# Another order of the four-pair start in an attention and two-layer feed-forward kernel

## The reference, cut to what matters

```
q_d, k_d, v_d = means over runs of 4 tokens            # 144 tokens a head
out_d     = softmax(q_d k_d^T / 8) v_d                  # then each row repeated 4 times
out_local = softmax(q k^T / 8 where |i - j| < 4) v      # a band of 7 keys for each query
x = (out_up + out_local) as 2304 tokens x 512
h = x @ w_in1;  x = max(0.01 h, h) @ w_out1
h = x @ w_in2;  return (h - tanh(h)) @ w_out2
```

## Time and profile before

| | us |
|---|---|
| median of three runs | 953.63 |
| lowest and highest | 953.53, 953.75 |
| the profiled execution, its own time | 953.53 |
| its span in the trace | 951.8 |
| PE busy | 939.1 (99%) |
| DVE, ACT, POOL busy | 541.2, 557.2, 403.1 |

### The profile page before, as it was taken

The page is one execution under the profiler, slowest core; times in us unless marked ns, Lnnn a source line. Parts: engine busy times, 40 slices in busy tenths (PEclk is TensorE's granted clock), DMA queues, the critical chain, the costliest instruction groups (busy, mean ns, idle before and its releaser), DMA issues.

```text
span 951.8 us, 19930 instructions
## 1 busy us (share of the span) xinstructions
PE 939.1 (99%) x7026; PEld 882.9 (93%) x7026; DVE 541.2 (57%) x1078; ACT 557.2 (59%) x1351; POOL 403.1 (42%) x343
## 2 busy tenths in 40 slices
PE   8999999999999999999999999999999999999998
PEld 7799999999999999999999989899899898898997
DVE  6755445534544554453236576776666766766764
ACT  4665546445446455463446687666666756756754
POOL 3685417327246155171533667332233233233232
PEclk9999999999999999999999999999999999999999
DMA  7875111210121121102004022000000000000000
GB/s 159 192 197 141 46 33 27 51 36 26 39 51 26 25 51 40 38 2 67 1 2 134 12 58 86 30 5 1 34 0 0 33 0 0 33 0 0 34 1 33
DMA packets 87797, 41.48 MB, mean 44 GB/s; under 512 B 60352, under 2 KB 81344, under 8 KB 87744
## 3 DMA queue, kind: packets, MB, share of 16 engines
q1 hardware_dynamic: 87744, 40.78, 16.3%
HBM read 36.04 MB, written 4.72 MB: 43 GB/s over the span
## 4 chain that ended last, share of the span: by engine, by line
PE 88%; ACT 3%; POOL 3%; DVE 2%; DMA 2%; issue 1%; SPq 0%; ACTq 0%; DVEq 0%; POOLq 0%
PE ph L538 13%; PE ph L539 13%; PE ph L540 13%; PE acc L567 7%; PE acc L568 7%; PE acc L569 7%; PE acc L614 6%; PE acc L615 6%; PE acc L616 6%; PE banks L427 2%; PE banks L464 2%; PE banks L451 1%; POOL g_lo L1149 1%; PE banks L420 1%; POOL w_lo_b L1156 1%
## 5 line engine op out<-in xcount | busy, mean ns | idle before, releaser
L1149 POOL TENSOR_TENSOR g_lo<-scratch,g_hi 128x384 fp32r<-128x384 f32 x96 | 125.6, 1309 | 257.8 <-ACT g_hi L741 257.8
L996 DVE TENSOR_TENSOR ph<-g,ph 128x288 f32<-128x288 f32 x128 | 59.0, 461 | 165.4 <-ACT g L755 164.7
L538 PE MATMUL ph<-x_hi,w_hi_a 128*128 128x288 f32 (+1 forms) x448 | 143.6, 321 | 0.4 <-DVE x_lo L978 0.2
L540 PE MATMUL ph<-x_hi,w_lo_a 128*128 128x288 f32 (+1 forms) x448 | 139.9, 312 | 0.0
L539 PE MATMUL ph<-x_lo,w_hi_a 128*128 128x288 f32 (+1 forms) x448 | 139.9, 312 | 0.0
L1128 POOL TENSOR_TENSOR in_lo<-w_whole,in_hi 128x512 fp32r<-128x512 f32 x64 | 82.4, 1287 | 134.7 <-ACT in_hi L721 133.9
L755 ACT ACTIVATE g<-ph 128x288 f32<-128x288 f32 x128 | 52.5, 410 | 136.3 <-PE ph L540 136.3
L1133 POOL TENSOR_TENSOR out_lo<-w_whole,out_hi 128x512 fp32r<-128x512 f32 x64 | 86.0, 1343 | 71.8 <-ACT out_hi L725 71.6
L1030 DVE SCALAR_TENSOR_TENSOR scratch<-scratch,ph 128x384 f32<-128x384 f32 x96 | 53.2, 554 | 108.6 <-ACT scratch L804 104.0
L803 ACT ACTIVATE scratch<-ph 128x384 f32<-128x384 f32 x96 | 46.8, 487 | 108.4 <-PE ph L540 106.9
L983 DVE TENSOR_TENSOR g_lo<-ph,g_hi 128x288 fp32r<-128x288 f32 x128 | 58.6, 458 | 59.2 <-ACT g_hi L741 59.2
(11 more groups left out here) (273 smaller groups left out, 2660.4 us busy)
## 6 DMA issues: line engine op xcount, KB each, us to landing
out_dram<-o_stage SPq DMA_DIRECT2D x18, 256.0 KB, 2.1
w_whole<-in_moe_w_in_dram SPq DMA_DIRECT2D x16, 256.0 KB, 4.2
w_whole<-in_moe_w_out_dram SPq DMA_DIRECT2D x16, 256.0 KB, 4.9
qn<-in_q_dram SPq DMA_DIRECT2D x26, 144.0 KB
kn<-in_k_dram SPq DMA_DIRECT2D x26, 144.0 KB
v4n<-in_v_dram SPq DMA_DIRECT2D x26, 144.0 KB
vw<-in_v_dram SPq DMA_DIRECT2D x26, 122.5 KB
scratch<-in_moe_w_in_dram SPq DMA_DIRECT2D x8, 256.0 KB, 2.8
```

The source lines that it names most:

```text
L538: pe.matmul(bank, whi, x_hi[:, c, 0:width], start=(c == 0), stop=False)
L540: last = pe.matmul(bank, wlo, x_hi[:, c, 0:width], start=False, stop=(c == CD - 1))
L996: dve.tensor_tensor(ph1[:, 1 - f % 2, 0:T1], g1[:, f % 2, :], ph1[:, 1 - f % 2, 0:T1], ALU.max)\
L1149: pool.tensor_tensor(g2_lo[:, f % 3, :], g2[:, f % 2, :], g2_hi[:, f % 3, :].bitcast(F32), ALU.subtract).then_inc(g_lo_done, 1)
```

## The change

The tables of exceptions of all four engines are changed, and the items between the steps are put at the beginning of a slot rather than behind a step. The order of the queues, from slot 4 on, comes out as follows (only what differs):

| engine | before | after |
|---|---|---|
| PE | B2 B3 A6; C2 C3 B6; D2 A14 D3 C6 D4 A15 B11 | B2 A6 B3; C2 B6 C3; D2 A14 C6 D3 A15 D4 B11 |
| ACT | C0 C1 A8; C3 B7 A11 D0 B8 A12; D3 C7 B11 C8 A15 B12; B14 D7 B15 | C0 A8 C1; C3 A11 B7 D0 A12 B8; D3 A15 B11 C7 B12 C8; B14 B15 D7 |
| ACT, items | D8 w0 C13 w1 D11 x0 C15 D13 x1 D15 x2 | D8 C13 w0 D11 C15 D13 w1 x0 x1 D15 x2 |
| DVE | B4 B5 A8 A9; C4 C5 B8 B9; D8 C12 D9 | B4 A8 B5 A9; C4 B8 C5 B9; D8 D9 C12 |
| DVE, items | D14 C16 D15 x0 x1 D16 x2 | D14 C16 x0 x1 D15 x2 D16 |
| POOL | A6 B6 A9 A10 B9; C6 C9 D6 C10 D9 D10 w0 w1 | A6 A9 A10 B6 B9; C6 C9 C10 D9 D10 D6 w0 w1 |

Here w0 and w1 are `split_kept(0)` and `split_kept(1)`, x0 to x2 the quarters of x. The dummy products stay with the same steps in the same number. No instruction is added or taken away.

```diff
-EARLY = 2
+KEPT_HI_SLOTS = (22, 26)
+KEPT_LO_SLOTS = (24, 27)
+FILL = {("a", 1): 2, ("a", 3): 2, ("b", 1): 1, ("b", 3): 2, ("c", 3): 2}
+X_HI_SLOTS = {27: (0, 1), 28: (2,)}
+X_LO_SLOTS = {27: (0, 1), 28: (2,)}
...
# PE
-            for step, s in batch0({(A, 6): (B, 3), (B, 6): (C, 3), (C, 6): (D4, 3), (A, 11): (C, 4), (A, 15): (D4, 4),
-                                   (B, 11): (D4, 4), (C, 15): (D4, 12), (C, 16): (D4, 14)}):
+            for _, step, s, i in batch0({(A, 11): (C, 4), (B, 11): (D4, 4), (C, 15): (D4, 12), (C, 16): (D4, 14)}):
...
# ACT
-            for step, s in batch0({(A, 8): (C, 1), (A, 11): (B, 7), (A, 12): (B, 8), (A, 15): (C, 8), (B, 11): (C, 7), (B, 12): (C, 8),
-                                   (D4, 7): (B, 14), (C, 15): (D4, 11)}):
-                attention(step, s, 0)
-                if (s, step) == (D4, 8):
-                    split_kept(0)
-                elif (s, step) == (C, 13):
-                    split_kept(1)
-                elif (s, step) == (D4, 11):
-                    split_first_x(0)
-                elif (s, step) == (D4, 13):
-                    split_first_x(1)
-                elif (s, step) == (D4, 15):
-                    split_first_x(2)
+            done = -1
+            for slot, step, s, i in batch0({(D4, 7): (B, 15), (C, 15): (D4, 11)}):
+                if slot != done:
+                    for c in X_HI_SLOTS.get(slot, ()):
+                        split_first_x(c)
+                if slot != done and kept_at(KEPT_HI_SLOTS, slot) is not None:
+                    split_kept(kept_at(KEPT_HI_SLOTS, slot))
+                done = slot
+                attention(step, s, i)
...
# DVE
-            for step, s in batch0({(A, 8): (B, 5), (B, 8): (C, 5), (C, 12): (D4, 8), (D4, 9): (C, 12),
-                                   (A, 15): (C, 14), (A, 16): (A, 15), (B, 15): (D4, 12), (B, 16): (B, 15),
-                                   (C, 15): (B, 16), (C, 16): (D4, 14)}):
-                attention(step, s, 0, 0, FIRST.index(s))
-                if (s, step) == (D4, 15):
-                    lo_of_first_x(0)
-                    lo_of_first_x(1)
-            lo_of_first_x(2)
+            done = -1
+            for slot, step, s, i in batch0({(C, 12): (D4, 9), (A, 15): (C, 14), (A, 16): (A, 15),
+                                            (B, 15): (D4, 12), (B, 16): (B, 15), (C, 15): (B, 16),
+                                            (C, 16): (D4, 14)}):
+                if slot != done:
+                    for c in X_LO_SLOTS.get(slot, ()):
+                        lo_of_first_x(c)
+                done = slot
+                attention(step, s, i, i, FIRST.index(s))
...
# POOL
-            for step, s in batch0({(B, 6): (A, 6), (D4, 6): (C, 9)}):
-                attention(step, s, 0)
-            for f in range(EARLY + 1):
-                split_kept(f)
+            done = -1
+            for slot, step, s, i in batch0({(D4, 6): (D4, 10)}):
+                if slot != done and kept_at(KEPT_LO_SLOTS, slot) is not None:
+                    split_kept(kept_at(KEPT_LO_SLOTS, slot))
+                done = slot
+                attention(step, s, i)
+            split_kept(EARLY)
```

More of the change, by code:

```diff
@@ L85, in two_scale_attention_and_feed_forward @@
     WHOLE = CF - KEPT
+    EARLY = len(KEPT_HI_SLOTS)
     assert D == QB and DM == CD * P and LP * RUN == S and NB * QB == S and PAIRS == 4 + 2 * MIXED
@@ L260, in batch0, with placed @@
         def batch0(behind):
-            def placed(at, s):
-                yield at, s
+            def placed(slot, at, s):
+                yield slot, at, s, 0
                 for (moved, step), place in behind.items():
                     if place == (s, at):
-                        yield from placed(step, moved)
+                        yield from placed(slot, step, moved)
             for slot in range(STEPS + 3 * BEHIND):
@@ L272, in batch0, with kept_at @@
                     if (s, at) not in behind:
-                        yield from placed(at, s)
+                        yield from placed(slot, at, s)
+        def kept_at(slots, slot):
+            return slots.index(slot) if slot in slots else None
         def later(f, tile, last):
@@ L636, in _ @@
             fill(8, ph1[:, 1, :])
-            fills = {(A, 1): 2, (A, 3): 2, (B, 1): 1, (B, 3): 2, (C, 3): 2}
-            for step, s in batch0({(A, 6): (B, 3), (B, 6): (C, 3), (C, 6): (D4, 3), (A, 11): (C, 4), (A, 15): (D4, 4),
-                                   (B, 11): (D4, 4), (C, 15): (D4, 12), (C, 16): (D4, 14)}):
-                attention(step, s, 0)
-                fill(fills.get((s, step), 0), ph1[:, 1, :])
+            for _, step, s, i in batch0({(A, 11): (C, 4), (B, 11): (D4, 4), (C, 15): (D4, 12), (C, 16): (D4, 14)}):
+                attention(step, s, i)
+                fill(FILL.get(("abcd"[FIRST.index(s)], step), 0), ph1[:, 1, :])
             for step in range(HEAD):
```

## The result

The changed kernel takes 959.66 us (median of four runs, 958.63 to 960.5) against 953.69: the ratio is 1.0062, 95% interval 1.0045 to 1.0080. It is slower, by 6.0 us; 957.4 was forecast, with 954.4 to 960.2 as the range. The four runs of before agreed within 0.3 us, those of after lie 1.9 us apart. The narrow spread of before did not last: in the 65 executions of it measured later, beside the experiments, it took 951.6 to 957.3 us and twice 964 us. The profiled execution of the changed kernel took 958.32 us, span 956.5: 4.8 us over that of before, one of the quicker ones.

What follows compares the result with a forecast made beforehand. PE bounds the kernel after 46.5 us, untouched; waits set the earlier part. 953.53 + 2.36 (-0.43 + 2.29 + 0.13 + 0.37) + 1.5 for one clock fall = 957.4 us, range 954.4 to 960.2.

Steps and rivals of the forecast that it cites:

- two falls or more: Rival: PE's clock falls at least twice, once right after the pause before `hidden1(0, 0)`; 958.9 to 960.5 us, chance 0.16.
- Step 1: PE, A6 before B3: A6 waits for DVE's L929, B's scores end later, DVE's B4 starts 0.54 us late.
- Step 2: DVE A8 before B5, POOL A9 before B6: POOL no longer delays L946 and L952; C3 leads by 1.6 us.
- Step 3: PE, B6 before C3: PE stands from 16.1 to 18.0 us; the lead at DVE's C4 is 1.4 us.
- Step 4: ACT, B7 behind A11: B's exponential waits for A11's eviction, DVE's B8 starts at 23.16; lead 0.7 us.
- Step 5: Around D4 on PE and ACT: C7 runs behind A15 and B11, DVE's C8 starts at 30.86, 0.4 us late.
- Step 6: DVE's D9, now ahead of C12, stands until POOL's product of D ends; POOL's D10 starts 0.43 us early.
- Step 7: POOL's D6 behind D10: weight blocks end later and delay DVE's low quarters; 2.29 us, plus 0.13 (D15) and 0.37 (x2).
- The clock: PE's clock falls to half around its pauses: one fall on C4's or D4's masks and scores, 1.5 us (0 to 4.5).
- no hold: Rival: POOL's weight blocks don't delay DVE's low quarters at the end of the start; 953.6 us, chance 0.13.
- faster: Rival: the 1.6 us lead at DVE's C3 survives, shown by C8 before 28.5 us; 951.3 us, chance 0.07.
- no fall: Rival: PE's clock does not drop to half on the critical path; 955.9 us, chance 0.24.

Runs made afterwards that it cites:

- after, again: The changed kernel, unaltered, measured and profiled a second time: 959.23 us against 953.75 for the kernel before, ratio 1.0066.
- B6 late alone: The kernel before with only POOL's three v sums of pair B moved from behind A6 to behind A10: 953.30 us against 953.81, ratio 0.9984.
- those with the dummies: The changed kernel plus dummy products on PE, seven behind C2 and eight ahead of `hidden1(0, 0)`: median 962.44 us, ratio 1.0072 to the kernel before.

## Why the prediction was right, and where it was off

The direction and the range held, and the profile shows the mechanism of the forecast: pauses of PE, exponentials queued behind evictions, the hold under the weight blocks. But the median is 2.3 us above the forecast and lies where the rival "two falls or more" had it (958.9 to 960.5, chance 0.16). The profile has two falls, the second in that rival's place. So the middle of the forecast was low, by two things: 0.7 us of waits ahead of D10, and too little time at half the clock.

- **Step 1** (A6 before B3): 0.54 us forecast, 0.93 measured (B4 at 15.47 for 14.54; A6 began at 11.93, not 11.78, and from there to the end of B's scores it took 3.51 us, not 3.27). Right in kind.
- **Step 2** (the hold of A goes): right. L948 0.17 and L954 0.20 us, C3 at 19.43 for 20.65, a lead of 1.2 where 1.6 was forecast.
- **Step 3** (PE waits for B5 before B6): the pause came, 1.62 us for 1.9. But C4 on DVE started at 23.40, 0.7 us late, where a lead of 1.4 was forecast. Of these 2.1 us the fall of the clock makes 1.37.
- **Step 4** (B7 behind A11): right. DVE waits 0.49 us before B8, and the single undoing of ACT's table gives 1.7 us of stretch back.
- **Step 5** (C7 behind A15 and B11): right. C8 waits 0.50 us for it. It starts at 32.84; 30.86 and one fall of 1.5 would be 32.36.
- **Step 6** (D9 under POOL's product of D): right in place (L954 1.05 us long, C14's pause 1.88 us), but D10 started at 40.34 where -0.43 + 1.5 on 38.57 gave 39.64. 0.7 us of this sum were missed: 0.4 of them in step 1; the rest is in steps 3 to 6 and isn't told apart. D8, which waits 1.22 us for ACT's D7, started at 37.45 where 35.3 and one fall gave 36.8.
- **Steps 1 to 6 together**: without a fall (after, again) it is 28.9 us from A's maxima to D10, 0.3 more than before, where the forecast had 0.4 less. B6 late alone in the kernel before makes it 25.4. So the gain from the hold of A is real, 3.2 us up to D10, and by difference the rest of the new order takes 3.5 us: more than all of it.
- **Step 7** (D6, the hold, x0 to x2): the term is 2.79 in the forecast (2.29 + 0.50) and 2.77 in the profile (10.63 - 7.86). The edit alone in the kernel before gives 2.74 and shows the cause. An agreement to 0.02 is luck, though: in the second profile, with its late fall, the piece is 4.4 us longer than before and the hold doesn't set it.
- **The clock**: one fall of 1.5 us on the path was taken. The one over C's scores costs 1.37 us (7.93 - 6.56), in the executions that have it. The second one of the first profile cost little: the last quarter waited for DVE and not for PE, and the part behind it is longer by 0.2 us, where the rival had 1.5. The low estimate is in the number and the length of falls: each of the nine profiles with the changed order on at least one of PE, DVE and ACT has one, five have two or three, and where it falls between 39 and 46 us it stays at half for 10 us and more, through the short products up to `hidden1`. Such long falls were not in the forecast. The granted clock of the timed executions fits: the changed kernel is at 0.996 in its quick ones (958.3, 958.6), at 0.993 or 0.994 in most and at 0.989 in its slowest (962.9).
- **A sign that failed**: "if the half clock lies on no scores, the time is 955.9". In the second profile it lies on none, and the time is 958.82: the late fall stretched step 7, and the waits ahead of D10 were 0.7 us more than forecast.
- **The rule of the Trainium skill weighed in the forecast** (TensorE: Matmul & The Clock Gate, Part 1) was right to be set aside: the clock did fall behind or in pauses of 1.3 to 3.0 us, though not in each execution, and once with no pause over 0.56 us in the 10 us before. **The rival "no hold"** is dead (0.41 us a quarter with POOL idle). **The rival "faster"** had its mark at C8 before 28.5 us; it came at 32.84. **The rival "no fall"** is 955.9; the two executions with a clock of 1.000 are those with the dummies, at 957.7 and 958.6.
- What I had wrong and the total didn't show: w1 "costs nothing". It makes POOL stand for 1.58 us right behind D6 once D6 is gone. So the terms don't add when taken away: D6 costs 2.3 us put into the kernel before, and taken out of the changed one it gives 0.6 us of stretch and nothing that the times show.

## What to carry to other kernels

When a start-up is bound by waits, carry each queue forward with the traced lengths and look at what stands ahead of each late item on every engine, the lightly busy ones too; that gave the place and the size of the largest term. Before an edit is undone to save its price, ask what is next in line: here it was w1 on ACT for POOL, and the slow clock for PE. And a pause of PE in a stretch of short products should be priced twice, once as the pause and once as the half clock that may follow it.

## What the runs showed of the hardware

- A DVE instruction with both inputs in SBUF, or a small scalar operation in SBUF, stood until a running POOL instruction was nearly over (2.98 us for 0.45; L954 1.05 us for 0.20). With POOL's next one ready it didn't get in between, though it had been waiting for 0.3 us. The same happened in each of the four profiles in which the first low quarter was issued under the first weight block: it was 2.98 to 4.05 us long. A maximum over PSUM (L941, 0.60 us at 20.95), a copy out of PSUM (L959, 0.66 at 40.18) or a sum over SBUF (L916, 1.49 at 19.43) beside POOL's work kept its length.
- The clock's fall isn't the same from run to run: C's scores took 1.66 us at 21.69 in one profile of the changed kernel, and in the other the interval around them was 1.37 us shorter. Once down between 39 and 46 us it stayed so for 10 to 14 us. In the second profile of the changed kernel PE was busy for all of the 10.30 us from 41.70 to 52.00, with 108 records of short products, transposes and products of `hidden1`, at half the clock throughout. In four of these five profiles it rose during `hidden1`, in the one with dummies during them (53.1); in one profile it also rose at 39.0, among short products.
